# Second routing's logits moved from TensorE to VectorE, Pool and ScalarE in a fused attention and two-layer expert kernel

## The chip, the cores and the metric

The kernel runs on one core of one Trainium2 chip. The metric is the device time of one execution in microseconds (us). The core's engines are TensorE (PE in the rows, its weight loads PEld), VectorE (DVE), ScalarE (ACT), GpSimd (POOL) and SyncE (SP); each runs its own instruction stream, and they meet at semaphores.

## The reference

Causal attention with forgetting, then two expert layers on its output. Each expert layer picks one of 8 experts for each of 2304 rows by the largest logit and scales that expert's output by the winning probability:

```python
# layer 2 (layer 1 takes normalised rows times normalised expert embeddings / tau as logits)
logits = x @ w_gate                      # x: output of layer 1, 2304 x 512; w_gate: 512 x 8
expert_idx = np.argmax(logits, axis=1)
probs = softmax(logits)
gate_w = probs[np.arange(N), expert_idx]
for e in range(E):
    xe = x[expert_idx == e]
    h = np.maximum(xe @ w1[e], 0.0)      # 512 -> 1024
    out[expert_idx == e] = gate_w[...] * (h @ w2[e])   # 1024 -> 512
```

## The kernel before

Attention runs over 32 heads in an order written out by hand. Beside it the first layer's routing is made, which fills a table in device memory: for each expert, in places of 128, the entries (row to gather, row to write, gate weight, place).

Then come two expert layers, m = 0 and m = 1, with the same code. For each expert a loop runs over its tiles of 128 rows (here 21 tiles in layer 0: experts have 2, 3, 3, 3, 2, 2, 3 and 3; 23 in layer 1). Each engine has its own copy of the loop, `tile_body`. All products are made in three passes, with high and low parts: hi by hi, hi weights' rest `wlo` by hi, and hi by the input's rest. One tile is:

- Pool gathers the rows (`rows_of`, L1212), TensorE turns them (L566), ScalarE makes `xT_hi` (L732), VectorE `xT_lo` (L1040). This runs one tile ahead.
- TensorE makes h in two halves (L559, 12 matmuls of 512 columns each). ScalarE does the first relu (L723) and the second (L728), TensorE turns h (L564, L572), ScalarE makes `hT_hi` (L730, L734), VectorE `hT_lo` (L1072, L1077).
- TensorE makes y (L588, 24 matmuls). VectorE copies the rows' numbers (`y_idx`, L1088) and scales y into `y_s` (L1089), and Pool stores it (`store_y`, L1228).

In an expert's first tile (`split`) ScalarE and VectorE also split the eight chunks of the next expert's weights, `whi` (L655, 128x1024) and `wlo` (L982), for the other of two buffers. They stand in two groups or more in the order of the tile: chunks 0 and 1, chunk 2 and up to 4, then 5 to 7.

Layer 0 also makes the second routing, for the y of the tile before. TensorE turns `y_s` (L570), ScalarE copies that to `xrT` (L650), TensorE makes the eight logits (L424, L581) and later the ranks (`ranks1`, L427). VectorE picks the expert (`route_choose`, L880, L886 to L904), ScalarE takes the exponentials (`route_exp`), and VectorE makes the entries of the table of layer 1 (`route_enter`, L910 to L927), which Pool scatters (`store_entries`, L1237). `link` (L757) makes VectorE wait for its own last instruction.

Every order is that of the code; a `wait_ge` stops its engine and everything behind it there. Pool's stream in a tile is: the next entries, their gather, the store of y, the store of the entries.

## Time and profile before

| | |
|---|---|
| median of 3 runs | 945.73 us (944.29 to 945.82) |
| the profiled execution | 944.56 us |
| its span, first to last instruction | 943.0 us |
| mean granted TensorE clock | 0.968 |
| busy: PE, PEld, DVE, ACT, POOL | 878.1, 722.4, 555.7, 403.5, 291.1 us |
| layer 0, first relu of the first to that of the last tile | 335.49 to 616.96 us |

The span is that of the profiled execution; the rows of its trace give starts in us from the span's beginning. Busy time of an engine that isn't waited for costs nothing, so what counts is the chain that sets the distance of one tile to the next.

### The profile page before, as it was taken

The numbers are of one execution on the slowest core, as the hardware profiler recorded it, in microseconds if no ns is written. First come the engines' busy times: TensorE is split into PE (matmuls) and PEld (weight loads), VectorE is DVE, ScalarE is ACT, GpSimd is POOL, SyncE is SP. The second block draws the span as 40 slices with busy tenths as digits, with TensorE's granted clock in tenths as the row PEclk, the third lists the DMA queues.
The fourth block names the chain that finished last, engine by engine and source line by source line (L and its number), as shares of the span: only waits on it lengthen the run. The fifth ranks groups of instructions, "written<-read, shape, count | busy, mean of one in ns | idle before, by whom it ended". The sixth has DMA issues, their size and how long they took to land.

```text
span 943.0 us, 16443 instructions
## 1 busy us (share of the span) xinstructions
PE 878.1 (93%) x5092; PEld 722.4 (77%) x5093; DVE 555.7 (59%) x1667; ACT 403.5 (43%) x708; POOL 291.1 (31%) x459
## 2 busy tenths in 40 slices
PE   6999988987988689999999999978999999999996
PEld 5787776766766568888888888867888888888884
DVE  6777674666766257675848874753554162626643
ACT  2554552553555045352625652614443242425542
POOL 6444334344332523222322322313212221122211
PEclk7999997998999899999999999999999999999998
DMA  4444442453530184543516642602565142616100
GB/s 130 112 116 114 123 119 64 142 160 95 143 111 13 29 299 163 177 136 115 184 59 213 213 170 86 216 20 90 197 216 184 46 150 102 211 46 217 39 30 23
DMA packets 59244, 119.64 MB, mean 127 GB/s; under 512 B 11934, under 2 KB 20638, under 8 KB 59204
## 3 DMA queue, kind: packets, MB, share of 16 engines
q1 hardware_dynamic: 49476, 96.90, 32.2%
q0 software_dynamic: 9440, 22.18, 7.2%
q8 instruction: 20, 0.33, 0.1%
q14 instruction: 20, 0.16, 0.1%
q10 hardware_dynamic: 288, 0.07, 0.0%
HBM read 104.14 MB, written 17.99 MB: 130 GB/s over the span
## 4 chain that ended last, share of the span: by engine, by line
PE 84%; DVE 4%; ACT 4%; DMA 3%; issue 2%; POOL 2%; SPq 1%; another core or an unknown queue 0%; POOLq 0%; DVEq 0%; ACTq 0%
PE ps L588 26%; PE ps L559 25%; PE ps L406 8%; PE ps L419 7%; PE ps L414 4%; PE ps L377 2%; PE ps L378 2%; PE ps L389 2%; PE ps L390 2%; PE ps L447 2%; PE ps L424 2%; ACT o_rows L638 1%; DMA xg<-x,ent_next 1%; PE ps L396 1%; DMA k_raw<-in_k 1%
## 5 line engine op out<-in xcount | busy, mean ns | idle before, releaser
L982 DVE TENSOR_TENSOR wlo<-stage,whi 128x1024 fp32r<-128x1024 f32 x136 | 160.0, 1220 | 31.6 <-ACT whi L655 26.0
L655 ACT CAST whi<-stage 128x1024 fp32r<-128x1024 f32 x136 | 133.7, 1055 | 0.1
L406 PE MATMUL ps<-probT,v_s 128*65 128x448 f32 (+4 forms) x384 | 109.2, 409 | 12.5 <-POOL probT L1143 12.4
L723 ACT ACTIVATE h_s<-ps 128x512 f32<-128x512 f32 x44 | 26.3, 599 | 220.5 <-PE ps L559 218.6
L823 DVE CUSTOM_DVE_ANT_0 ps<-ps,maskf 128x576 f32<-128x576 f32 (+4 forms) x160 | 76.1, 508 | 51.6 <-PE ps L378 51.6
L588 PE MATMUL ps<-whi,hT_hi 128*128 128x512 f32 x352 | 100.5, 408 | 0.0
L588 PE MATMUL ps<-whi,hT_lo 128*128 128x512 f32 x352 | 99.2, 403 | 0.0
L559 PE MATMUL ps<-whi,xT_hi 128*128 128x512 f32 x352 | 95.1, 392 | 3.0 <-DVE xT_lo L1040 3.0
L588 PE MATMUL ps<-wlo,hT_hi 128*128 128x512 f32 x352 | 95.2, 393 | 0.0
L559 PE MATMUL ps<-whi,xT_lo 128*128 128x512 f32 x352 | 95.1, 392 | 0.0
L559 PE MATMUL ps<-wlo,xT_hi 128*128 128x512 f32 x352 | 94.7, 391 | 0.0
L624 ACT ACTIVATE probT<-ps 128x576 f32<-128x576 f32 (+4 forms) x160 | 66.2, 435 | 53.1 <-PE ps L390 49.3
L389 PE MATMUL ps<-qB,kB 97*128 97x288 f32 (+2 forms) x192 | 72.4, 385 | 10.6 <-ACT probT L624 10.6
L559 PEld LDWEIGHTS ps<-whi,xT_hi 128*128 128x128 f32 x352 | 65.7, 188 | 18.1 <-ACT xT_hi L714 3.5
L588 PEld LDWEIGHTS ps<-wlo,hT_hi 128*128 128x128 f32 x352 | 66.6, 189 | 14.9
L559 PEld LDWEIGHTS ps<-wlo,xT_hi 128*128 128x128 f32 x352 | 66.1, 188 | 14.6
L559 PEld LDWEIGHTS ps<-whi,xT_lo 128*128 128x128 f32 x352 | 66.1, 188 | 14.4
L1072 DVE TENSOR_TENSOR hT_lo<-ps,hT_hi 128x512 fp32r<-128x512 f32 x44 | 30.4, 690 | 73.1 <-ACT hT_hi L730 72.9
L588 PEld LDWEIGHTS ps<-whi,hT_hi 128*128 128x128 f32 x352 | 63.3, 190 | 11.3
L588 PEld LDWEIGHTS ps<-whi,hT_lo 128*128 128x128 f32 x352 | 63.0, 188 | 11.7
L406 PEld LDWEIGHTS ps<-probT,v_s 128*65 128x65 f32 x384 | 47.1, 143 | 28.8 <-issue 17.0
L1216 POOL COPY ent_next<-ent_tab 128x4 int32 (+1 forms) x46 | 8.5, 186 | 193.5 <-DVE ent_mid L1041 191.6
(188 smaller groups left out, 1582.3 us busy)
## 6 DMA issues: line engine op xcount, KB each, us to landing
stage<-in_moe_w SPq DMA_DIRECT2D x128, 512.0 KB, 3.7
q_raw<-in_q SPq DMA_DIRECT2D x64, 144.0 KB, 3.1
k_raw<-in_k SPq DMA_DIRECT2D x64, 144.0 KB, 3.1
v_s<-in_v SPq DMA_DIRECT2D x32, 162.5 KB, 2.2
x<-o_rows SPq DMA_DIRECT2D x8, 512.0 KB
kB<-cum_hl SPq DMA_DIRECT2D x64, 2.2 KB, 1.8
table<-entry POOLq DMA_INDIRECT x44, 2.1
table<-tinit SPq DMA_DIRECT2D x2, 288.0 KB
```

What stands on the lines that cost most here:

```text
L389: pe.matmul(o, kB[a][0:ROW + 1, k0:k0 + P], qB[a][0:ROW + 1, lo:hi], start=True, stop=False)
L406: mm = pe.matmul(ps[0:D + 1, OT_AT + lo:OT_AT + hi], v_s[h % 3][:, t, :], probT[:, col:col + hi - lo], start=(t == 0), stop=(t == QT - 1 o ...
L414: mm = pe.matmul(back_ps[:, t, :], o_t[:, t * P:(t + 1) * P], i_emb[:, h % H, :], start=True, stop=True)
L419: mm = pe.transpose(bank[:, c * P:(c + 1) * P], src[:, c * P:(c + 1) * P], ident[:])
L559: mm = pe.matmul(h_ps[hf], x[:, c * P:(c + 1) * P], w1_sl(w[b], c, hf * 512, 512), start=(wi == 0 and c == 0), stop=(wi == 2 and c == DC - 1))
L588: mm = pe.matmul(y_ps, h[:, kk * P:(kk + 1) * P], w2_sl(w[b], kk), start=(hf == 0 and wi == 0 and kk == 0), stop=(hf == 1 and wi == 2 and ...
L624: act.activation(probT[0:M, PT_AT[t]:PT_AT[t] + S - t * P], ps[0:M, T_AT[t]:T_AT[t] + S - t * P], ACT.Exp, scale=-1.0).then_inc(exps_done, 1)
L655: act.copy(whi[b][:, c, :], stage[:, c, :]).then_inc(w_hi[c], 1)
L723: act.activation(h_s[:, 0:512], h_ps[0], ACT.Relu).then_inc(h_relu[0], 1)
L823: dve.tensor_tensor_reduce(out=tile, in0=tile, in1=maskf[0:M, at:at + q1], scale=1.0, scalar=LARGE, op0=ALU.add, op1=ALU.min, accum_out=sm ...
L982: dve.tensor_tensor(wlo[b][:, c, :], stage[:, c, :], whi[b][:, c, :].bitcast(F32), ALU.subtract).then_inc(w_lo[c], 1)
L1072: dve.tensor_tensor(hT_lo[:, 0:512], hT_ps[0], hT_hi[:, 0:512].bitcast(F32), ALU.subtract).then_inc(h_lo[0], 1)
```

## The change

In layer 0 the turn of `y_s`, the copy `xrT` and the eight logits on TensorE go. The logits come from products of `y_s` with the gate's rows, which a new input brings broadcast over all partitions (`wg_rows`, 128 x 8 x 512, loaded by SP before head 16). For experts 0 to 2 VectorE multiplies and sums (`first_logits`); for 3 to 7 Pool multiplies (`products`) into two buffers in turn, and ScalarE sums (`accumulate`). The scale of y goes from VectorE to ScalarE and waits for `y_placed`, the copy of `y_idx`. On VectorE the entries of a tile's choice are made one tile later, ahead of the next choice, with `ent_prev` for the rows' numbers, and so the ranks on TensorE too, between the two halves of h. In split tiles ScalarE splits chunks 0 and 1 ahead of the first relu, not behind it. After the last tile the last logits are still made on TensorE, as before, and there is one pass of entries more. Layer 1 is as it was.

```diff
@@ TensorE, tile
                                 mm.then_inc(h_done[hf], 1)
+                                if m == 0 and hf == 0:
+                                    pe.wait_ge(oh_done, tile.get(1, B - 1))
+                                    ranks1().then_inc(rank_done, 1)
                             yr = tile.get(1, 1 + 2 * m)
                             pe.wait_ge(y_ready, yr)
-                            if m == 0:
-                                turn_rows(y_s, yT_ps).then_inc(r_turned, 1)
...
-                                    if wi == 2 and m == 0 and hf == 0:
-                                        pe.wait_ge(rT_ready, tile.get(1, 1))
-                                        pe.wait_ge(ent_done[1], tile.get(1, 1))
-                                        logits(wg_s, rt_lg).then_inc(logits_done, 1)
-                                    if wi == 2 and m == 0 and hf == 1:
-                                        pe.wait_ge(oh_done, tile.get(1, B))
-                                        ranks1().then_inc(rank_done, 1)
@@ ScalarE
+            def accumulate(i, k):
+                act.wait_ge(prod_done, k)
+                act.activation(prod[i % 2][:], prod[i % 2][:], ACT.Copy,
+                               accum_out=lg[:, 0, NV + i:NV + i + 1]).then_inc(acc_done, 1)
...
                 act.copy(xT_hi[:], x_ps).then_inc(x_hi, 1)
+                if m == 0:
+                    for i in range(NP):
+                        accumulate(i, i + 1)
@@ ScalarE, tile
+                            if split and m == 0:
+                                for c in range(0, 2):
+                                    split_hi(1 - b, c, nw)
                             act.wait_ge(h_done[0], n)
                             act.activation(h_s[:, 0:512], h_ps[0], ACT.Relu).then_inc(h_relu[0], 1)
...
+                            if m == 0:
+                                for i in range(2):
+                                    accumulate(i, tile.get(NP, i + 1))
                             act.wait_ge(h_done[1], n)
                             act.activation(h_s[:, 512:1024], h_ps[1], ACT.Relu).then_inc(h_relu[1], 1)
...
                             if m == 0:
-                                route_turned(tile.get(1, 1), yT_ps)
+                                for i in range(2, NP):
+                                    accumulate(i, tile.get(NP, i + 1))
...
                                 route_exp(tile.get(1, B))
+                                act.wait_ge(y_done, n)
+                                act.wait_ge(y_placed, n)
+                                act.activation(y_s[:], y_ps, ACT.Copy,
+                                               scale=ent_cur[:, 2:3].bitcast(F32)).then_inc(y_ready, 1)
@@ VectorE
+            def first_logits():
+                for i in range(NV):
+                    ins = dve.tensor_tensor_reduce(out=yT_ps, in0=y_s[:], in1=wg_rows[:, i, :], scale=1.0, scalar=0.0,
+                                                   op0=ALU.mult, op1=ALU.add, accum_out=lg[:, 0, i:i + 1])
+                    link(ins)
@@ VectorE, tile
                             if split:
                                 for c in range(0, 2):
                                     split_lo(1 - b, c, nw)
+                            if m == 0:
+                                first_logits()
...
+                            if m == 0:
+                                route_enter(rank_n, ex_n, out_n, one_rk, one_ent)
+                                link(dve.tensor_copy(ent_rt[:], ent_prev[:]))
                             if split:
                                 split_lo(1 - b, 2, nw)
                             if m == 0:
-                                route_choose(1, tile.get(), one_rt)
+                                dve.wait_ge(acc_done, acc_n)
+                                route_choose()
                             if split:
                                 for c in range(3, 5):
                                     split_lo(1 - b, c, nw)
...
+                            if m == 0:
+                                dve.wait_ge(y_out, out_n)
+                                dve.tensor_copy(y_idx[:], ent_cur[:, 1:2]).then_inc(y_placed, 1)
@@ Pool
+            def products(n):
+                for i in range(NP):
+                    pool.wait_ge(acc_done, tile.get(NP, 1 - NP + n) if i == 0 else tile.get(NP, i - NP + n))
+                    pool.tensor_tensor(prod[i % 2][:], y_s[:], wg_rows[:, NV + i, :], ALU.mult).then_inc(prod_done, 1)
...
                             store_y(m, tile.get(1, 2 * m) if m else n)
                             if m == 0:
+                                products(0)
                                 store_entries(n)
```

ScalarE, an expert's first tile in layer 0, before. `h_s` is the relu, `ISA` stands for waits on a register.

```order
L723 ACTIVATE h_s<-ps 128x512
L654 ISA
L655 CAST whi<-stage 128x1024 x2
L728 ACTIVATE h_s<-ps 128x512
L730 CAST hT_hi<-ps 128x512
```

And now, from the split of chunks 0 and 1 to the second relu:

```order
L657 CAST whi<-stage 128x1024 x2
L731 ACTIVATE h_s<-ps 128x512
L242 ISA
L651 ACTIVATE prod,lg<-prod 128x512
L242 ISA
L651 ACTIVATE prod,lg<-prod 128x512
L739 ACTIVATE h_s<-ps 128x512
```

Two sums now stand between the two relus, and the two splits ahead of the first.

The end of the same tile on ScalarE, now, from the third sum on:

```order
L651 ACTIVATE prod,lg<-prod 128x512
L657 CAST whi<-stage 128x1024 x3
L242 ISA
L646 ACTIVATE ex<-lgm 128x8
L756 ACTIVATE y_s<-ps,ent_cur 128x512
L657 CAST whi<-stage 128x1024 x3
```

The scale of y, which waits for VectorE, stands ahead of the last three splits.

Pool, one tile, now (before, only the copy, the two DMAs and the DMA of the entries stood there):

```order
L1264 COPY ent_next<-ent_tab 128x4
L239 ISA
L1272 DMA xg<-x,ent_next 128x512
L1281 DMA y<-y_s,y_idx 2305x512
L242 ISA
L1289 TENSOR_TENSOR prod<-y_s,wg_rows 128x512
L242 ISA
L1289 TENSOR_TENSOR prod<-y_s,wg_rows 128x512
```

The products (five in all, the last three follow in the same way) stand between the store of y and that of the entries.

## Rows read from the trace of the kernel before

**Rows 1.** Waits, 330 to 640 us: who waited for whom, total, times, longest.
```profile
POOL y L1233 <- DVE y_s L1089: 111.3, 21, 11.4
```

**Rows 2.** ScalarE's first relus in order of time: start, duration, idle before.
```profile
335.49 0.60 ACT L723 ACTIVATE h_s<-ps 128x512 f32<-128x512 f32 x1 [3.90 <-PE ps L559]
...
353.98 0.60 ACT L723 ACTIVATE h_s<-ps 128x512 f32<-128x512 f32 x1 [3.00 <-PE ps L559]
...
616.96 0.60 ACT L723 ACTIVATE h_s<-ps 128x512 f32<-128x512 f32 x1 [5.84 <-PE ps L559]
...
675.51 0.60 ACT L723 ACTIVATE h_s<-ps 128x512 f32<-128x512 f32 x1 [7.63 <-PE ps L559]
...
687.95 0.60 ACT L723 ACTIVATE h_s<-ps 128x512 f32<-128x512 f32 x1 [1.96 <-PE ps L559]
```

**Rows 3.** TensorE in order of time, an ordinary tile of layer 0.
```profile
403.45 1.07 PE L588 MATMUL ps<-whi,hT_hi 128*128 128x512 f32 x4
...
404.36 1.08 PE L588 MATMUL ps<-wlo,hT_hi 128*128 128x512 f32 x4
...
406.37 1.12 PE L559 MATMUL ps<-whi,xT_hi 128*128 128x512 f32 x4
```

**Rows 4.** Groups of VectorE by form: count, busy us, mean ns, idle before.
```profile
L823 DVE CUSTOM_DVE_ANT_0 ps<-ps,maskf 128x448 f32<-128x448 f32 x32 | 20.4, 639 | 9.6 <-PE ps L378 9.5
L823 DVE DVE_READ_ACCUMULATOR2_ANT smin<- 128x1 fp32r x128 | 18.0, 141 | 0.0
```

**Rows 5.** ScalarE in order of time, activations with accumulator.
```profile
111.92 0.62 ACT L638 ACTIVATE o_rows<-o_rows 128x512 f32<-128x512 f32 x1
...
112.53 0.62 ACT L638 ACTIVATE o_rows<-o_rows 128x512 f32<-128x512 f32 x1
```

**Rows 6.** Pool in order of time, a copy.
```profile
248.38 0.66 POOL L1136 CAST kB<-kA 64x576 fp32r<-64x576 f32 x1 [4.43 <-DVE kA L783]
```

**Rows 7.** Pool and VectorE in order of time, a copy beside a two-input instruction.
```profile
242.36 1.16 POOL L1131 CAST qB<-qA 64x576 fp32r<-64x576 f32 x1 [0.27 <-ACT qA L618]
...
242.25 0.75 DVE L795 TENSOR_TENSOR kA<-k_raw,kB 64x576 fp32r<-64x576 f32 x1
```

**Rows 8.** In order of time, layer 1's first tile from the second relu.
```profile
653.39 0.60 ACT L728 ACTIVATE h_s<-ps 128x512 f32<-128x512 f32 x1 [0.26 <-PE ps L559]
...
654.52 1.20 PE L588 MATMUL ps<-whi,hT_hi 128*128 128x512 f32 x4
...
655.77 0.68 DVE L1077 TENSOR_TENSOR hT_lo<-ps,hT_hi 128x512 fp32r<-128x512 f32 x1
```

**Rows 9.** VectorE in order of time: entries, the next tile, an expert's first tile.
```profile
393.58 0.16 DVE L914 COPY entry<-ent_rt 128x2 int32<-128x2 int32 x1
...
396.11 0.17 DVE L1067 COPY ent_cur<-ent_mid 128x4 int32<-128x4 int32 x1 [0.56 <-DVE ent_rt L1093]
...
411.14 0.17 DVE L1067 COPY ent_cur<-ent_mid 128x4 int32<-128x4 int32 x1 [1.77 <-issue]
```

**Rows 10.** In order of time, the middle of an expert's first tile.
```profile
415.91 1.23 DVE L982 TENSOR_TENSOR wlo<-stage,whi 128x1024 fp32r<-128x1024 f32 x1 [0.24 <-ACT whi L655]
...
417.05 0.15 DVE L886 TENSOR_SCALAR valid<-ent_rt 128x1 f32<-128x1 int32 x1
...
417.82 2.93 ACT L655 CAST whi<-stage 128x1024 fp32r<-128x1024 f32 x3
...
418.70 2.35 DVE L982 TENSOR_TENSOR wlo<-stage,whi 128x1024 fp32r<-128x1024 f32 x2
```

**Rows 11.** In order of time, the scale of y and Pool's store of it.
```profile
406.76 0.74 DVE L1089 TENSOR_SCALAR y_s<-ps,ent_cur 128x512 f32<-128x512 f32 x1
...
408.36 1.01 POOL L1233 DMA_INDIRECT y<-y_s,y_idx  x1 [5.18 <-DVE y_s L1089]
```

**Rows 12.** Layer 0's first tile: TensorE's turn of the gathered rows, then a window.
```profile
341.47 0.66 PE L419 MATMUL ps<-ident,xg 128*128 128x128 f32 x4 [2.83 <-DMA xg<-x,ent_next]
...
343.00:345.00 2.00, 2.00 (x7) 1.61 (x7) 1.24 (x3) 1.54 (x3) 0.28 (x2) 0.50 1.04 408
```

More of the change, by code:

```diff
@@ L40, in attention_moe_moe @@
     HALF = H // 2
+    NV = 3
+    NP = E - NV
     SCALE = -float(D) ** -0.5
@@ L166, in attention_moe_moe @@
         y_idx = sb("y_idx", [P, 1], I32)
+        ent_prev = sb("ent_prev", [P, 4], I32)
+        prod = [sb(f"prod{a}", [P, DM]) for a in range(2)]
+        wg_rows = sb("wg_rows", [P, E, DM])
         ps = ctx.enter_context(nc.psum_tensor("ps", [P, 8 * 512], F32))
@@ L317, in _ @@
             for h in range(HEADS):
+                if h == 2 * H:
+                    sp.dma_start(wg_rows[:].rearrange("p e d -> p (e d)"), wg_t).then_inc(wg_in, 16)
                 if h + 2 < HEADS:
@@ L420, in turn_rows, with logits @@
                 return mm
-            def logits(w, o, rows=xrT):
+            def logits(w, o, rows):
                 for c in range(DC):
@@ L706, in _ @@
                 else:
-                    act.wait_ge(ent_out, tile.get(16, 32))
+                    act.wait_ge(ent_out, tile.get(16, 48))
                     act.wait_ge(tab_in[0], 16 * E // 2)
@@ L748, in _ @@
                 if m == 0:
-                    route_turned(tile.get(1, 1), yT_ps)
+                    act.wait_ge(r_turned, 1)
+                    act.copy(prod[0][:], yT_ps).then_inc(rT_ready, 1)
                     route_exp(tile.get(1, B))
@@ L894, in route_choose @@
                 link(dve.tensor_reduce(first_i[:, lo:lo + g], e, AX.X, ALU.min))
-                if m == 0:
-                    link(dve.tensor_tensor(first_i[:, lo:lo + g], first_i[:, lo:lo + g], pad_row[:], ALU.add))
-                    dve.tensor_tensor(oh[:, lo:lo + g, :], e, wide(first_i, lo, g), ALU.is_equal).then_inc(oh_done, 1)
-                else:
-                    dve.tensor_scalar(oh[:, 0, :], e[:, 0, :], first_i[:, 0:1], valid[:, 0:1], ALU.is_equal,
-                                      ALU.mult).then_inc(oh_done, 1)
@@ L901, in route_choose @@
-                dve.tensor_scalar(region[:, lo:lo + g], first_i[:, lo:lo + g], float(TOK), float(E * TOK), ALU.mult, ALU.add)
-                if m == 1:
-                    link(dve.tensor_scalar(inval[:], valid[:], -float(OOB), float(OOB), ALU.mult, ALU.add))
-                    dve.tensor_tensor(region[:, 0:1], region[:, 0:1], inval[:], ALU.add)
+                link(dve.tensor_tensor(first_i[:, lo:lo + g], first_i[:, lo:lo + g], pad_row[:], ALU.add))
+                dve.tensor_tensor(oh[:, lo:lo + g, :], e, wide(first_i, lo, g), ALU.is_equal).then_inc(oh_done, 1)
@@ new lines, in route_choose_batch, with route_choose @@
+                dve.tensor_scalar(region[:, lo:lo + g], first_i[:, lo:lo + g], float(TOK), float(E * TOK), ALU.mult, ALU.add)
+            def route_choose():
+                l, e = lg[:, 0:1, :], eqi[:, 0:1, :]
+                dve.tensor_scalar(valid[:], ent_rt[:, 3:4], float(E * TOK), None, ALU.is_lt)
+                link(dve.tensor_reduce(mx[:, 0:1], l, AX.X, ALU.max))
+                link(dve.tensor_tensor(e, l, wide(mx, 0, 1), ALU.is_equal))
+                dve.tensor_tensor(lgm[:, 0:1, :], l, wide(mx, 0, 1), ALU.subtract).then_inc(lgm_done, 1)
+                link(dve.scalar_tensor_tensor(out=e, in0=e, scalar=-float(E), in1=iota8[:].unsqueeze(1), op0=ALU.mult,
+                                              op1=ALU.add))
+                link(dve.tensor_reduce(first_i[:, 0:1], e, AX.X, ALU.min))
+                dve.tensor_scalar(oh[:, 0, :], e[:, 0, :], first_i[:, 0:1], valid[:, 0:1], ALU.is_equal,
+                                  ALU.mult).then_inc(oh_done, 1)
+                dve.tensor_scalar(region[:, 0:1], first_i[:, 0:1], float(TOK), float(E * TOK), ALU.mult, ALU.add)
+                link(dve.tensor_scalar(inval[:], valid[:], -float(OOB), float(OOB), ALU.mult, ALU.add))
+                dve.tensor_tensor(region[:, 0:1], region[:, 0:1], inval[:], ALU.add)
@@ L1278, in _ @@
                     if m == 0:
+                        if late == 0:
+                            products(0)
                         store_entries(tile.get(1, late))
@@ L1281, in _ @@
                     store_entries(tile.get(1, 2))
+                    store_entries(tile.get(1, 3))
             pool.wait_ge(y_out, tile.get(16, 48))
@@ L1306 @@
     }
+    gate = np.asarray(inputs['moe2_w_gate'])
     for name in ('moe_w1', 'moe_w2', 'moe2_w_gate', 'moe2_w1', 'moe2_w2'):
         laid_out[name] = np.asarray(inputs[name])
+        if name == 'moe2_w_gate':
+            laid_out['gate_rows'] = np.broadcast_to(gate.T.reshape(1, -1), (P, gate.size))
     arrays, args = {}, []
```

89 lines of the change are left out of this document (47 added, 42 removed).

## The prediction

> **What bounds the kernel now.** Start with the page's busy shares and the waits of the first expert layer. TensorE is busy almost without a break, and the large waits there are those of others for it or for what follows it: Pool stands 111 us for y_s [rows 1]. Next come the starts of the first relu. The first layer's 20 intervals are one of 18.49 and 19 of 13.84 (353.98 to 616.96); in the second layer they are 12.44 [rows 2]. A tile of the first layer is a tile of the second plus the turn of y, the logits and the ranks. TensorE sets both periods, so removed TensorE work is worth its full time until something else takes longer than the shorter tile.
>
> **What leaves TensorE.** The two periods differ by 1.40. The rank matmuls stay. Two groups of four matmuls with the ranks between them take 2.01 (404.36 to 406.37), where one group alone takes 0.91 [rows 3]; so the ranks cost 0.19. The rest, 1.21 a tile, goes. TensorE alone could run a tile in 12.6.
>
> **What each new step costs.**
> - Three multiply-and-sum instructions on VectorE. The same custom instruction takes 0.64 at 448 wide [rows 4], about 0.70 at 512; with its accumulator read (0.14, mostly overlapped) and the wait that links each to the next I take 0.9. Three are 2.7 a tile.
> - Five sums on ScalarE. A 512-wide activation with accumulator starts 0.61 to 0.62 after the one before [rows 5]. Five are 3.1, and the y scale adds 0.5 to 0.6, while the xrT copy of that size goes.
> - Five products on Pool. No row shows this. One 576-wide copy of one SBUF operand takes 0.66 [rows 6], or 0.58 at 512: the lower bound. Two operands through that rate are 1.15, which I take; the copy that ran beside a two-input VectorE instruction took 1.16 [rows 7], so a product can reach 1.8 with such a delay. On this price alone a page has more: the Trainium skill, "GPSIMD Engine Reference", section 3.1, measures 2.6 cycles an element at 1.2 GHz for a two-tensor add, from which I would estimate 1.1 us, and no run here shows it.
>
> **The new ring.** These steps are harmless only if they stay off the path, and the order written out doesn't let them. ScalarE does the second relu, which TensorE needs for its turn of h and thus for all of the second product, only after sums 0 and 1. These need Pool's products 0 and 1, which come after Pool's store of the last y, which waits for ScalarE's scale, which waits for VectorE's y_idx. And y_idx now stands behind the three logits, the entries, all five sums and the choice. I count from the start of one second relu to the next.
>
> *Ordinary tile.* The second layer shows the second hT_lo on VectorE 2.38 after the relu (653.39 to 655.77), for 0.68 [rows 8]. The entries took 1.98 (393.58 to the end of the 0.37 copy before the idle of 0.56) [rows 9]: 5.2 with a short wait. The choice took 1.65 (417.05 to 418.70) [rows 10], less about 0.1 for the lg copy that goes: 6.8. y_idx 0.15: 7.0. TensorE has y done at 1.13 + 6 x 0.91 + 0.3 = 6.9 [rows 8], so y_idx is last, by a little. ScalarE's scale: 7.6. Pool starts its store 0.86 after y_s and takes 1.01 [rows 11]: 9.5. Two products and gaps of 0.35: 12.15. Sum 1: 12.8. So with no collision 12.8 stands against TensorE's 12.6 and today's 13.84. The three logits run from about 8.0 to 10.7, and product 0 starts at 9.8; if they collide it costs up to 0.7, and at an expert's end Pool also loads a table (up to 1). I take 13.6, between 12.6 and 14.2.
>
> *Into an expert's first tile.* ScalarE must walk the loop's head, where VectorE showed 1.77 of idle time [rows 9] (ScalarE's own was hidden; I take 1.7), then split two chunks before the first relu, 0.98 each (2.93 for three) [rows 10]: 7.6 + 1.7 + 1.96 = 11.3. First relu 0.5, two sums 1.24: 13.0. VectorE's two wlo chunks run from about 10.3 to 12.6, in front of the logits. If product 1 has to wait for them, 14.4.
>
> *Out of that tile.* This is the costly one. VectorE: wlo 0 and 1 end near -0.4 (against the relu), logits 2.3, hT_lo and xT_lo 4.4, entries 6.4, wlo 2 (1.2) 7.6, choice 9.1, wlo 3 and 4 (2.35 [rows 10]) 11.4, y_idx 11.6. Today y_idx stands behind wlo 4 too, but with no logits and no entries ahead of it, and ScalarE doesn't wait for it. Now ScalarE stands before its scale until 11.6, with splits 5 to 7 queued behind: 0.5 + 2.95 gives 15.05; then first relu and two sums, 16.8. TensorE, which wanted the relu at 12.6, idles about 4 us. Pool is worse off if it collides: y_s at 12.2, store to 14.0, and product 0 at 14.3 meets wlo 6 and 7. With two products behind them it is 19 to 20.3.
>
> So the pair of intervals around a first tile takes 13.0 + 16.8 = 29.8 with no collision, 14.4 + 20.3 = 34.7 with all, against 27.7 now. The rows show one such collision: a Pool copy that takes 0.66 alone took 1.16 when a VectorE tensor_tensor with two SBUF inputs started 0.11 before it [rows 7]. The wait was partial, and who goes first isn't shown. I take the middle, 32.2: +4.5.
>
> The Trainium skill says more than the row ("SBUF — State Buffer", section "Who interferes with whom"): a VectorE instruction with two SBUF inputs and a Pool instruction that reads SBUF exclude each other for the whole instruction, by order of issue. By it the sum would be nearer 34.7, and it speaks against giving both engines products of y at once.
>
> **Start, end, and what is free.** At the start Pool's first round of products is on a zero y, and products 2 to 4 wait for ScalarE's sums, which come after xT_hi. So the second gather goes out about 4 later, into full DMA engines. TensorE already waited 2.83 for it, and ran at half of its clock, 0.50, behind that [rows 12]. I take +6 (3 to 8). At the end there is one more pass of entries, 2.0, partly beside TensorE's work: +1.5 (0 to 3). The 2 MB load of wg_rows stands in SP's queue at head 16, ahead of head 18's operands, two heads early; I cost it at nothing, and up to 3 if that cover is gone. Gathers go out after product 4, some 3 us later than now; behind the first tile TensorE waits for no gather in this layer, so I cost that at nothing, and at up to 2 a tile if the cover is less than that. The ranks, moved between the halves of the first product, read a choice made one tile ago: nothing. Each long idle of TensorE may cost 1 to 1.5 in clock, as in rows 12, up to +10 in all; that is for the range.
>
> **Sum.** 7 pairs x 4.5 = +31.5; 5 ordinary intervals x -0.24 = -1.2; start +6; end +1.5: +37.8. The profiled execution took 944.56, 1.17 less than the median of 945.73; 944.56 + 37.8 + 1.17 is 983.5, and I say 983.
>
> **Rivals.**
> 1. Collisions cost nothing and Pool is quick: pairs 29.8 (+14.7), ordinary 12.8 (-5), start +4: 959. For it: the partial wait in rows 7. Chance 0.2.
> 2. Every collision is a full wait, as the page says: pairs 34.7 (+49), ordinary 14, start and end +8: 1003. Chance 0.2.
> 3. Faster: products and sums are always ready, TensorE sets the tile, 19 x -1.21 with +3 at the start: 926. It decides at y_idx of a first tile: that would have to stand some 4 us earlier than I have it. Against it are VectorE's rows, which sum to 11 us without a gap. But ordinary tiles could gain, and first tiles lose less than I think: 0.12.
> 4. The two cancel, within 0.2%: 0.03.
>
> My forecast, part of the collisions, has 0.45. The range of 950 to 1006 takes in rivals 1 and 2 and leaves out the third. A measurement can tell about 0.2% here: faster 0.12, same 0.03, slower 0.85.
>
> **What would show it.** In the changed profile, starts of the first relu should alternate: about 17 to 18 behind an expert's first tile, 13 to 14 elsewhere. ScalarE should wait for y_idx in first tiles, and TensorE for h_s. A Pool product should take 1.1 to 1.2 alone and longer beside wlo. If TensorE's turn of h never waits, I am wrong and it is rival 3; if products take 0.6, rival 1.

## The result, and the profile after

The changed kernel takes 1074.34 us (median of 4 runs, 1071.67 to 1075.73) against 945.38 for the kernel before (median of 4, 944.29 to 945.82): a ratio of 1.136, 95% interval 1.134 to 1.139. The forecast was 983, in a range of 950 to 1006. The direction was right, the size was not: +129 us, where +38 was forecast.

The page of the kernel after, with its busy shares, the chain of work that ended last, and four of its groups (line, engine, operation, count, then busy us, mean ns, idle before it and what ended that):

```profile
PE 919.4 (86%) x4842; PEld 735.6 (68%) x4843; DVE 707.5 (66%) x1787; ACT 479.0 (45%) x928; POOL 449.5 (42%) x570
...
PE 51%; DVE 19%; issue 15%; ACT 6%; POOL 4%; DMA 3%; SPq 1%; DVEq 1%; ACTq 1%; POOLq 0%
...
L1008 DVE TENSOR_TENSOR wlo<-stage,whi 128x1024 fp32r<-128x1024 f32 x136 | 218.9, 1653 | 45.4 <-ACT whi L657 44.7
L1289 POOL TENSOR_TENSOR prod<-y_s,wg_rows 128x512 f32<-128x512 f32 x110 | 159.2, 1475 | 18.0 <-ACT prod L651 17.4
L586 PE MATMUL ps<-whi,hT_lo 128*128 128x512 f32 x352 | 109.0, 436 | 48.1 <-DVE hT_lo L1110 48.0
...
L1001 DVE CUSTOM_DVE_ANT_0 ps<-y_s,wg_rows 128x512 f32<-128x512 f32 x63 | 84.2, 1336 | 1.9
```

TensorE's share fell from 93% to 86%, and TensorE now waits 48 us for `hT_lo`, a wait that it did not have. A `wlo` of 128x1024 took 1.23 in the rows of before [rows 10]; its mean is now 1.65 us, over all 136. The logits' instruction (L1001) has a mean of 1.34, where alone it takes 0.70.

ScalarE's first relus, the rows that answer to [rows 2], are those of the layer's first tile, the next two, its last tile and the first of layer 1:

```profile
343.82 0.59 ACT L731 ACTIVATE h_s<-ps 128x512 f32<-128x512 f32 x1
...
368.17 0.59 ACT L731 ACTIVATE h_s<-ps 128x512 f32<-128x512 f32 x1
...
386.82 0.59 ACT L731 ACTIVATE h_s<-ps 128x512 f32<-128x512 f32 x1
...
741.10 0.60 ACT L731 ACTIVATE h_s<-ps 128x512 f32<-128x512 f32 x1 [2.06 <-PE ps L564]
...
781.83 0.60 ACT L731 ACTIVATE h_s<-ps 128x512 f32<-128x512 f32 x1 [3.91 <-PE ps L564]
```

Three differences hold all of it. The first relu came 8.3 us later than before (335.49). The stretch from it to the last tile's, which I call **the stretch** from here on, is 397.3 us where it was 281.5: +115.8. From there to layer 1's first relu it is 40.7 instead of 33.7: +7.0. Together +131.1, and the two profiled executions differ by 131.2 (1075.73 and 944.56). Layer 1's period is 12.4 in both. The layer's first interval needs care: it was 18.49 before and is 24.35 now, and in the kernels of the experiments it lies anywhere between 16.7 and 25.3. Without it the stretch is 263.0 before and 372.9 now, +110.0.

Inside the stretch the 20 intervals alternate as forecast, but all of them are long. Out of an expert's first tile they are 22.3 to 22.8 (the very first 24.35), ordinary ones 18.5 to 18.8. Into a first tile they are 16.0 to 16.4 behind an expert of three tiles and 18.6 to 19.5 behind one of two.

The waits of the kernel after from 330 to 760 us (who waited for whom, us in total, times, longest):

```profile
ACT ex L646 <- DVE lgm L916: 101.3, 21, 6.1
...
PE ps L586 <- DVE hT_lo L1110: 48.0, 15, 4.9
...
ACT y_s L756 <- DVE y_idx L1130: 28.9, 13, 3.1
PE ps L426 <- ACT h_s L739: 26.9, 17, 2.5
...
DVE entry L934 <- DMA table<-entry: 16.5, 7, 5.0
```

The two waits that I had forecast are there: `y_s` for `y_idx`, and the turn of h for the second relu (L426 for L739). The largest of TensorE's is a third, for `hT_lo`, which stood in no step of mine. Where it comes from is seen in order of time, first in an ordinary tile, then in an expert's first tile:

```profile
427.94 5.63 DVE L1001 CUSTOM_DVE_ANT_0 ps<-y_s,wg_rows 128x512 f32<-128x512 f32 x1
427.98 5.03 POOL L1289 TENSOR_TENSOR prod<-y_s,wg_rows 128x512 f32<-128x512 f32 x4
...
443.53 6.30 DVE L1008 TENSOR_TENSOR wlo<-stage,whi 128x1024 fp32r<-128x1024 f32 x1 [0.54 <-ACT whi L657]
443.79 4.96 POOL L1289 TENSOR_TENSOR prod<-y_s,wg_rows 128x512 f32<-128x512 f32 x4
...
455.08 2.07 PE L586 MATMUL ps<-whi,hT_lo 128*128 128x512 f32 x4 [4.91 <-DVE hT_lo L1110]
...
456.95 1.91 PE L586 MATMUL ps<-whi,hT_hi 128*128 128x512 f32 x4
```

One instruction of VectorE that needs 0.70 lasts 5.63 while Pool runs four products in 5.03, and one that needs 1.2 lasts 6.30. Each has a record that starts ahead of the first product's. VectorE is let in only when Pool stands still, waiting for a sum of ScalarE's. Everything that is queued on VectorE behind it comes late, `hT_lo` among it. TensorE, done with its two passes on `hT_hi`, waits 4.91 us for that, and its next groups of four matmuls take 2.07 and 1.91 us where they take 1.1 to 1.2 at full clock. The granted clock is 0.50, the lower of TensorE's two levels (1.2 of 2.4 GHz), from 455 to 459 us, behind that wait, and 1.00 again from 461. From 353 to 629 us its mean is 0.85, and 1.00 before.

In the layer's second tile it is otherwise. A `wlo` had begun 0.96 us ahead of the first product, it took its 1.23, and then the two engines went by turns:

```profile
366.40 1.23 DVE L1008 TENSOR_TENSOR wlo<-stage,whi 128x1024 fp32r<-128x1024 f32 x1 [1.75 <-ACT whi L657]
367.36 1.39 POOL L1289 TENSOR_TENSOR prod<-y_s,wg_rows 128x512 f32<-128x512 f32 x1
...
368.72 2.24 POOL L1289 TENSOR_TENSOR prod<-y_s,wg_rows 128x512 f32<-128x512 f32 x1
...
369.76 2.28 DVE L1008 TENSOR_TENSOR wlo<-stage,whi 128x1024 fp32r<-128x1024 f32 x1
```

Of the 21 rows of products from the layer's first tile to its last, 13 shut an instruction of VectorE out and 8 went by turns. Whether an instruction is shut out depends on who came first, if Pool's coming is put about 0.74 us ahead of where its record starts. Nine kernels of this document have rows of Pool instructions that read SBUF: this one and those of experiments 3, 4, 7 to 10, 12 and 13. In them 391 VectorE instructions with two SBUF inputs start within 1.2 us ahead of the first record of a row or just with it. All 140 that start at most 0.73 us ahead are shut out. None of the 241 that start 0.745 us or more ahead lasts longer than alone. Of the 10 between, 3 are shut out. In the 8 rows with turns a `wlo` was still running when the first product's record started, and that product took 1.39 to 1.46: there Pool was the one that had to wait first.

### The profile page after: what moved, and what is told of

Read it like the earlier page. It is cut to its first block, busy times and chain, and to the rows that moved or that the text cites. A ratio compares the mean times of both kernels' runs of the same rounds, so it can differ in the third digit from the quotient of the medians.

```text
span 1074.1 us, 16623 instructions
## 1 busy us (share of the span) xinstructions
PE 919.4 (86%) x4842; PEld 735.6 (68%) x4843; DVE 707.5 (66%) x1787; ACT 479.0 (45%) x928; POOL 449.5 (42%) x570
## 4 chain that ended last, share of the span: by engine, by line
PE 51%; DVE 19%; issue 15%; ACT 6%; POOL 4%; DMA 3%; SPq 1%; DVEq 1%; ACTq 1%; POOLq 0%
PE ps L586 16%; PE ps L564 12%; PE ps L413 7%; DVE wlo L1008 7%; PE ps L421 3%; PE ps L426 3%; POOL prod L1289 2%; PE ps L384 2%; ACT whi L657 2%; PE ps L385 2%; PE ps L396 2%; DMA table<-entry 2%; PE ps L397 2%; DVE ps L1001 1%; ACT o_rows L638 1%
## 5 line engine op out<-in xcount | busy, mean ns | idle before, releaser
L1008 DVE TENSOR_TENSOR wlo<-stage,whi 128x1024 fp32r<-128x1024 f32 x136 | 218.9, 1653 | 45.4 <-ACT whi L657 44.7
L1289 POOL TENSOR_TENSOR prod<-y_s,wg_rows 128x512 f32<-128x512 f32 x110 | 159.2, 1475 | 18.0 <-ACT prod L651 17.4
L586 PE MATMUL ps<-whi,hT_hi 128*128 128x512 f32 x352 | 121.2, 475 | 0.0
L586 PE MATMUL ps<-wlo,hT_hi 128*128 128x512 f32 x352 | 106.9, 430 | 0.0
L651 ACT ACTIVATE prod<-prod 128x512 f32<-128x512 f32 x110 | 69.4, 635 | 51.6 <-POOL prod L1289 51.2
L426 PE MATMUL ps<-ident,h_s 128*128 128x128 f32 x352 | 59.3, 295 | 37.4 <-ACT h_s L739 26.9
L586 PEld LDWEIGHTS ps<-wlo,hT_hi 128*128 128x128 f32 x352 | 77.0, 219 | 19.6
L586 PEld LDWEIGHTS ps<-whi,hT_hi 128*128 128x128 f32 x352 | 76.8, 229 | 15.3
L1001 DVE CUSTOM_DVE_ANT_0 ps<-y_s,wg_rows 128x512 f32<-128x512 f32 x63 | 84.2, 1336 | 1.9
L426 PEld LDWEIGHTS ps<-ident,h_s 128*128 128x128 f32 x352 | 42.3, 149 | 53.9 <-issue 31.2
```

The costliest lines, as they stand in the source:

```text
L426: mm = pe.transpose(bank[:, c * P:(c + 1) * P], src[:, c * P:(c + 1) * P], ident[:])
L586: mm = pe.matmul(y_ps, h[:, kk * P:(kk + 1) * P], w2_sl(w[b], kk), start=(hf == 0 and wi == 0 and kk == 0), stop=(hf == 1 and wi == 2 and ...
L651: act.activation(prod[i % 2][:], prod[i % 2][:], ACT.Copy, accum_out=lg[:, 0, NV + i:NV + i + 1]).then_inc(acc_done, 1)
L1001: ins = dve.tensor_tensor_reduce(out=yT_ps, in0=y_s[:], in1=wg_rows[:, i, :], scale=1.0, scalar=0.0, op0=ALU.mult, op1=ALU.add, accum_out= ...
L1008: dve.tensor_tensor(wlo[b][:, c, :], stage[:, c, :], whi[b][:, c, :].bitcast(F32), ALU.subtract).then_inc(w_lo[c], 1)
L1289: pool.tensor_tensor(prod[i % 2][:], y_s[:], wg_rows[:, NV + i, :], ALU.mult).then_inc(prod_done, 1)
```

## The experiments

The measure is the time and, since parts of the computation are left out in some kernels (which changes the tiles of layer 1), the stretch. All but the twelfth have one execution each. The kernel before took 943 to 950 us beside them, and the first interval of the stretch moves by some us from kernel to kernel, so differences of a few us prove little.

**Theory A:** Pool's products keep VectorE out of a resource that both need to reach SBUF, for a whole row of products, and that is what the time went to. **Theory B:** the new orders do it, the ring from y through products, sums and choice back to the scale of y, whatever Pool's instructions are.

**1. Pool busy as long, but it only writes.**

```diff
-                    pool.tensor_tensor(prod[i % 2][:], y_s[:], wg_rows[:, NV + i, :], ALU.mult)
+                    pool.memset(wide_prod[i % 2][:], 0.0)        # 128x1370
```

> Each of Pool's five products per tile is replaced by a memset of 1370 columns into the same buffer (about 1.25 us by the size, as a product alone): Pool is busy as long and signals as often, but reads nothing from SBUF. The logits of experts 3 to 7 are therefore zero sums and layer 1's tiles differ, so layer 0 is judged by the stretch from the first to the last first relu (281.5 us before, 397.3 after); wg_rows holds three experts only. Theory A (Pool's tensor_tensor products, run back to back, keep VectorE's two-input instructions out; hT_lo comes late, TensorE waits and its clock falls): the stretch falls to about 310 us (295 to 330), no wlo or logits instruction is longer than 1.6 us for one of its size, and TensorE's waits for hT_lo (48 us) fall under 10. Theory B (the longer ring itself: Pool's time, the sums between the relus, the scale of y behind the exponential): the stretch stays within 15 us of 397, since Pool's times and all orders are the same.

Measured: 1046.64 us, stretch 348.4. The line of `wlo` and that of the memsets in this kernel (count, then shortest/median/longest in ns):

```profile
L1009 DVE TENSOR_TENSOR wlo<-stage,whi x136: 1215/1219/1227, 247.1 to 1038.9; 128x1024 fp32r<-128x1024 f32 x136
...
L1291 POOL MEMSET prod<- x110: 1240/1257/1279, 328.3 to 694.4; 128x1370 f32 x110
```

No `wlo` is lengthened any more, though 38 of layer 0's 64 stand beside a memset, and TensorE's waits for `hT_lo` fall from 48.0 to 4.2 us in all. The stretch is 48.9 us shorter. Both theories missed the number: A is right on the cause of the long instructions, but what is left is 67 us above before, not 30.

**2. No Pool work.** The memsets have one column.

> Pool's products are one-column memsets, so Pool's time goes too, and all signals, sums and orders stay (logits of experts 3 to 7 are zero sums; layer 0 is judged by its stretch of relus). Theory A: as the kernel with write-only products, 295 to 325 us, at most 10 us under it, since Pool's time alone is hidden. Theory B with Pool's time in the ring: well under the kernel with write-only products, by 20 us or more. If it is the orders on ScalarE and VectorE that cost, it stays above 360.

Measured: 1014.80 us, stretch 319.1, so 29.3 less than with the long memsets. That is more than the 10 of theory A and what B had asked for (20 or more). It does not tell Pool's time in the ring from a hold by its writes, which experiments 5 and 14 show. Of the 115.8 us, 78.2 go with Pool's work and 37.6 stay: these are the orders. The wait of `entry` for the store of the tile before, right ahead of the choice and of `y_idx`, is now 45.7 us in 22 times: 1.5 to 3.0 each, and 5.1 once, behind the last tile.

**3. The whole changed kernel with an early scale.**

```diff
@@ ScalarE, tile
-                                route_exp(tile.get(1, B))
                                 act.wait_ge(y_done, n)
                                 act.wait_ge(y_placed, n)
                                 act.activation(y_s[:], y_ps, ...)
                             if split:
                                 for c in range(5, CH):
                                     split_hi(1 - b, c, nw)
+                            if m == 0:
+                                route_exp(tile.get(1, B))
@@ VectorE, tile: y_idx and y_placed right behind the second hT_lo, ahead of route_enter
```

> The full changed kernel with the copy of the rows' numbers right behind the second hT_lo on VectorE, and with ScalarE's scale of y ahead of the exponential and the splits of chunks 5 to 7 ahead of the exponential too. Theory A: the products are still there and still shut VectorE out for whole runs; they only start earlier, so the stretch of layer 0 stays between 375 and 400 us (397.3) and the time between 1050 and 1077. Theory B (the late scale closes a ring y, products, sums, choice): the scale moves up by 3 to 4 us a tile, the stretch falls under 345 us and the time under 1025.

Measured: 1046.28 us, stretch 384.0: 13.3 less, inside A's range for the stretch and far from B's. The time gains 28 and falls below A's range for it, because this execution also reached its first relu 13.5 us earlier (below) and lost 2.8 less between the layers.

**4. The other way round: the kernel before, with products that nobody needs.**

```diff
                             store_y(m, tile.get(1, 2 * m) if m else n)
                             if m == 0:
+                                for i in range(5):
+                                    pool.tensor_tensor(out5[i][:], dum[0][:], dum[1][:], ALU.mult)
                                 store_entries(n)
```

> The kernel before, with five tensor_tensor products of 128x512 on Pool in each tile of layer 0 behind the store of y, on tiles that nobody else uses and with nobody waiting for them; all of the computation is as before. Theory A: VectorE's two-input instructions (wlo, hT_lo, xT_lo) are kept out by up to 6 us a tile; the stretch of layer 0 grows from 281.5 to between 305 and 345 us and TensorE waits for hT_lo. Theory B: Pool has the time free (its busy share is low), nobody waits, the stretch stays under 285 us.

Measured: 1067.35 us, stretch 395.5. Nothing but these products was added, no engine waits for them, and they cost 114.0 us of stretch: as much as the whole change. VectorE's group of `scum`, the running sum of the choices, in layer 0 (busy us, mean ns), and one tile in order of time:

```profile
L928 DVE TENSOR_TENSOR scum<-scum,oh 128x8 bf16<-128x8 bf16 x20 | 126.3, 6314 | 0.0
...
438.56 6.99 DVE L928 TENSOR_TENSOR scum<-scum,oh 128x8 bf16<-128x8 bf16 x1
...
439.23 6.28 POOL L1278 TENSOR_TENSOR out<-dum 128x512 f32<-128x512 f32 x5
...
450.84 2.07 PE L590 MATMUL ps<-whi,hT_lo 128*128 128x512 f32 x4 [4.12 <-DVE hT_lo L1074]
```

An addition of 8 columns that takes 0.15 lasts 6.99, from 0.67 us ahead of the first product's record to the end of the fifth. TensorE's wait of 4.12 and its slow matmuls behind it (2.07, 1.91 and 1.64 for groups of 1.1 to 1.2, at a granted clock of 0.50 from 450.8 to 454.8 us) make 6.4 of the 6.9 by which this tile is longer than 13.83. B falls as the main cause, and A stands, but not with its number or its instructions: it had 305 to 345, and `wlo`, `hT_lo` and `xT_lo` kept out. `wlo` keeps its 1.22 here and `hT_lo` its 0.69; the one shut out is tiny, and they stand behind it.

**5 and 6. The early scale, with Pool only writing, and with no Pool work.**

> Write-only Pool work (memsets of 1370 columns in place of the products, so the logits of experts 3 to 7 are zero sums and layer 0 is judged by its stretch of relus) together with the early scale of y. Reads of the products were worth 48.9 us of that stretch (397.3 against 348.4) and the early scale 13.3 us (397.3 against 384.0). If the two add up, it is 335 us. If the early scale was worth so little only because the kept-out VectorE set the tile (theory A), it is worth more here, 25 to 45 us: 303 to 323 us. If the late scale never mattered, 345 to 350.

> One-column memsets in place of the products (logits of experts 3 to 7 are zero sums) together with the early scale: what is left is the order on ScalarE and VectorE alone. The stretch of layer 0 was 319.1 us with the late scale. If the late scale and the entries' wait ahead of it cost the pairs, 285 to 295 us (tiles of 12.4 to 14.4); if the two early splits, the sums between the relus and VectorE's longer row do, it stays over 305 us.

Measured: 1050.53 us with a stretch of 350.3, and 997.77 us with 302.6. The fifth missed: no gain at all over the first (348.4), though the sixth shows that the early scale has something to give. With the scale earlier the memsets stand beside the choice, and its last steps now last as long as a row of memsets. In order of time:

```profile
357.47 4.88 DVE L922 TENSOR_SCALAR oh<-eqi,first_i,valid 128x8 bf16<-128x8 f32 x1
357.53 4.79 POOL L1291 MEMSET prod<- 128x1370 f32 x4
```

So Pool's writes shut VectorE out too, but other instructions of it; experiment 14 comes back to this. The sixth lies between its two readings, nearer to the second: the early scale is worth 16.5 us when nothing is in VectorE's way (319.1 to 302.6).

**7. One SBUF input on Pool in place of two:** in the fourth kernel, `pool.tensor_copy(out5[i][:], dum[:])` of 128x1024.

> The kernel before with five copies of 128x1024 (one SBUF input) on Pool per tile of layer 0 in place of the five added products, about 1.2 us each; all of the computation is as before. With products one tiny two-input instruction of VectorE (scum, L928, 128x8) took 6.3 us a tile. Theory A1 (any Pool instruction that reads SBUF keeps it out): again 5 to 7 us a tile there, the stretch of layer 0 between 380 and 400 us. Theory A2 (only Pool instructions with two inputs): L928 takes under 1.5 us and the stretch is under 290 us.

Measured: 1022.50 us, stretch 356.5. The copies take 1.04 us each, and `scum` has this group:

```profile
L928 DVE TENSOR_TENSOR scum<-scum,oh 128x8 bf16<-128x8 bf16 x20 | 91.3, 4563 | 0.0
```

A copy shuts VectorE out like a product (median of `scum` 5.65 us, and five copies last 5.0). The stretch is under my 380; that the row is 1.3 us a tile shorter explains most of it.

**8. A memset of 300 columns behind each product.**

> The kernel before with the five added products per tile, each followed by a write-only memset of 300 columns (about 0.3 us) on Pool; both inputs of a product are one tile; all of the computation is as before. If the waiting VectorE instruction gets in as soon as no reading Pool instruction runs, scum (L928) takes 0.2 to 1.8 us instead of 6.3 and the stretch of layer 0 falls from 395.5 to under 310 us. If VectorE is let in only when Pool stops or after a fixed number, it takes 5 us or more and the stretch stays over 375 us.

Measured: 1060.44 us, stretch 393.7. One row of the spaced kernel, in order of time:

```profile
437.64 6.88 DVE L929 TENSOR_TENSOR scum<-scum,oh 128x8 bf16<-128x8 bf16 x1
438.31 1.05 POOL L1278 TENSOR_TENSOR out<-dum 128x512 f32<-128x512 f32 x1
439.29 0.36 POOL L1279 MEMSET gap<- 128x300 bf16 x1
...
444.44 0.34 POOL L1279 MEMSET gap<- 128x300 bf16 x1
```

A memset as such does not stop `scum`: in experiment 14 it stands as close ahead of a row of memsets (0.63 to 0.68 us in 18 of 19 tiles) as here ahead of the products, and keeps its 0.15. Yet gaps of 0.35 us with memsets in them let nothing in. While instructions follow each other on Pool, it keeps the way.

**9. A pause behind each product:** Pool waits for its own product before it issues the next.

```diff
                                     pool.tensor_tensor(out5[i][:], dum[0][:], dum[1][:], ALU.mult).then_inc(pch, 1)
                                     chain.add()
+                                    pool.wait_ge(pch, chain.get())
```

> The kernel before with the five added products per tile, and behind each of them Pool waits for its own product to be done before it issues the next, so that it stands still for a part of a microsecond, in which a memset stood in the spaced kernel. All of the computation is as before. If the port is handed over only when Pool has nothing under way, scum (L928) now gets in behind the first or second product and takes 1 to 3 us instead of 6.3, and the stretch of layer 0 falls from 395.5 to between 282 and 320 us. If VectorE is let in only behind the last of a fixed row of Pool instructions, whatever the gaps, it takes 7 us or more and the stretch is over 390 us.

Measured: 1034.62 us, stretch 362.6. In order of time:

```profile
436.79 2.03 DVE L928 TENSOR_TENSOR scum<-scum,oh 128x8 bf16<-128x8 bf16 x1
437.47 1.32 POOL L1278 TENSOR_TENSOR out<-dum 128x512 f32<-128x512 f32 x1
438.97 1.33 POOL L1278 TENSOR_TENSOR out<-dum 128x512 f32<-128x512 f32 x1 [0.18 <-POOL out L1278]
...
441.92 3.46 DVE L984 TENSOR_TENSOR wlo<-stage,whi 128x1024 fp32r<-128x1024 f32 x2
441.94 2.36 POOL L1278 TENSOR_TENSOR out<-dum 128x512 f32<-128x512 f32 x1 [0.18 <-POOL out L1278]
```

`scum` gets in behind the first product (2.03 us): a pause of 0.18 does what a memset of 0.35 did not. But the stretch gained only 32.9 us, not 75 or more. Two long rows now go by turns: `wlo` has a mean of 1.74 and a product one of 1.57, and Pool's row lasts longer and meets 38 of the layer's `wlo` where in experiment 4 it met one.

**10. The same pause in the changed kernel with the early scale.**

> The changed kernel with the early scale, and Pool waits for each of its products to be done before it issues the next. The whole computation is there. The stretch of layer 0 was 384.0 us with the early scale alone, and 302.6 with the early scale and no products at all. If standing still lets VectorE in, wlo and the logits' instructions take 2.4 us at most and the stretch falls to 320 to 350 us; if Pool's own time in the ring (products, sums, choice) is what is left, the pauses make it longer, 385 to 400 us.

Measured: 1053.68 us, stretch 382.6, so 1.4 less than without the pauses. The longest `wlo` is 2.92 us where it was 6.64, but the mean of the logits' instruction is 1.28 in both. It does not help here: the collisions are cut into pieces, not removed, and my 320 to 350 was wrong.

**11 and 12. Entries staged in a tile of their own**, without products and with them, both with the early scale.

```diff
             def route_enter(n, n_ex, n_out, ranks, ent):
-                dve.wait_ge(ent_out, n_out)
                 dve.tensor_copy(ent[:, 0, 0:2], ...)          # ent is now entry2
...
+                dve.wait_ge(ent_out, n_out)
+                link(dve.tensor_copy(entry1[:], entry2[:]))
                 dve.sem_inc(ent_done[1], 1)
```

> The kernel without products and with the early scale (layer 0: 302.6 us, then 38.8 us to the first relu of layer 1), in which VectorE makes an entry in a tile of its own and copies it into the one that Pool stores only at the end, so that the wait for the store of the tile before comes some 2 us later and at the end of the row. Logits of experts 3 to 7 are zero sums. If this wait (39.5 us in 22 tiles) is on the path, the stretch falls to 285 to 293 us and the stretch between the layers to 33 to 36 us; if not, both stay within 2 us.

> The changed kernel with the early scale and with the staged entries, whole computation, products in place. Without products these two brought layer 0 to 283.7 us; with products and the early scale alone it was 384.0. If the products' hold on the port is what costs, they still cost 80 to 100 us here: 365 to 384 us, and the gap between the layers is about 36 us. If products only cost as long as the other orders are bad, it is under 330 us.

Measured: without products 976.76 us and a stretch of 283.7, 18.9 less than in the sixth kernel. With products 1044.97 us (ratio to before 1.106, interval 1.099 to 1.113) and a stretch of 381.1. So with the orders mended the products cost 97.5 us, more than in the kernel as changed: their price is not the orders' doing. And all of this change with products at no cost (283.7) is not shorter than the kernel before (281.5).

**13. One product per tile on the kernel before.**

> The kernel before with one added product per tile of layer 0 instead of five; all of the computation is as before. Five cost 114 us of the stretch of layer 0 (281.5 to 395.5). If every product has its share of that (scum is kept out for one product, 1.3 us more, and all of it is on the path), the stretch is 295 to 305 us; if VectorE has slack for one, 281 to 286 us.

Measured: stretch 285.4 (time 940.45, with an early first relu). `scum` lasts 2.0 us in most tiles (median 2026 ns), and 3.9 us are lost in 20 intervals. The first of them happens to be 1.8 shorter than before (16.7); the other 19 lose 5.7 us, where with five products they lose 111.8. So five cost some twenty times what one does: VectorE had room for one wait of 1.9, not for one of 6.8.

**14. Memsets on the kernel before.**

> The kernel before with five memsets of 128x1370 (about 1.25 us each) per tile of layer 0 in place of the five added products: Pool writes and reads nothing; all of the computation is as before. Two-input instructions (scum, L928, and wlo) should keep their 0.16 and 1.22 us. If only reads cost, the stretch stays between 281 and 290 us. But in an earlier run copies and tensor_scalars of VectorE grew beside memsets to 5.7 us; if such a one stands there in most tiles (the copy of ent_rt or ent_cur), the stretch is 340 to 395 us as with products.

Measured: 1031.57 us, stretch 374.2, inside the range for the case that a copy stands there. In order of time:

```profile
439.99 0.15 DVE L927 TENSOR_TENSOR scum<-scum,oh 128x8 bf16<-128x8 bf16 x1
...
440.29 6.36 DVE L1094 COPY ent_rt<-ent_cur 128x4 int32<-128x4 int32 x1
...
440.64 5.98 POOL L1272 MEMSET out<- 128x1370 bf16 x5
```

Here it is the copy of 4 columns behind `scum` that lasts 6.36. In the fourth kernel it was `scum`, and the copy behind it, 0.17 us, came when Pool had finished.

## Why the prediction failed, step by step

The direction and the order of the long and short intervals came as forecast. In the forecast's own terms the seven pairs took 40.0 each where it had 32.2 (+85.9 in place of +31.5), and the five ordinary intervals 18.6 where it had 13.6 (+24.1 in place of -1.2). The start is +14.2 in place of +6, the end +7.0 in place of +1.5. One step carries most of it.

- **TensorE's part, right.** Without Pool's work (experiment 2) ordinary intervals are 12.2 to 13.1; I had 12.6 for TensorE alone. No run shows the ring's 12.8 free of collisions with Pool's time in it: with the long memsets an ordinary interval is 14.1.
- **Prices of one instruction, right but for the product.** Three logits start 0.79 apart (426.35, 427.14, 427.94), taken as 0.9. Sums start 0.62 apart (433.10 and 433.72), taken as 0.62. A product takes 1.25 to 1.30 alone, where I took 1.15. The estimate of 1.1 from the Trainium skill, "GPSIMD Engine Reference", section 3.1, was a little lower still. The median of the 105 products in experiment 4 is 1.29.
- **The failed step: what a collision costs.** I wrote of the ordinary tile that the logits run beside product 0 and "if they collide it costs up to 0.7", and I took the middle between no collision and one wait. What stands there is 5.63 for 0.70, +4.9. The step had two faults. It counted the wait of one instruction for one other, where VectorE waits for the whole row of products up to Pool's next pause. And it priced it at the colliding instruction and at Pool, when VectorE's `hT_lo` stands behind it and TensorE's last pass behind that. An expert of three tiles (into, out and an ordinary interval) was forecast at 32.2 + 13.6 = 45.8, and at 48.7 with every collision a full wait. It took 57.3 (16.4, 22.3 and 18.7), 46.8 without Pool's work, 41.5 before. So my second rival failed too, for the same reason: 1003 against 1074.
- **The row it was judged by.** [rows 7] showed one Pool copy that took 1.16 instead of 0.66 beside a VectorE instruction. There Pool was the one that waited, and only one instruction of it stood there: the row could show neither what a series does nor that VectorE can be the one shut out, though I did write that who goes first isn't shown.
- **The published rule.** The Trainium skill, "SBUF — State Buffer", section "Who interferes with whom", has a VectorE instruction with two SBUF inputs and a reading Pool instruction exclude each other for a whole instruction, and has it depend on who issues first. That there is a full block, and that reads make it for `tensor_tensor` and writes do not, is what experiments 1, 4 and 14 show. That the order decides agrees too, with Pool's coming some 0.74 us ahead of its record (140 of 140 and 241 of 241, above). The length does not agree where Pool was first: in these runs it goes on over four and five instructions. I held this rule as a rival only, and even its price of one instruction was far too low.
- **Orders without collisions, too low by 28.** Rival 1, pairs of 29.8 and ordinary intervals of 12.8, makes a stretch of 291 with the first interval as it was; experiment 2 has 319.1. Of the 28, 4.7 are in that first interval and belong to the start; the pairs are 33.3. What I left out is the wait of `entry` for the store of the tile before, 1.5 to 3.0 us in each tile (moved to the end of its row in experiment 11, it gave back 18.9). I had "5.2 with a short wait". The late scale, which I did name, is worth 16.5.
- **Clock.** I let up to 10 us for it in the range and nothing in the sum. In the tile of experiment 4 three groups of matmuls behind the stall of 4.12 took 2.3 us more than at full clock. Were it so in each of 20 tiles it would make 46 us, an estimate of mine from that one tile.
- **Start, +6 forecast, +14.2 measured.** The forecast's start was the late second gather, and that came as told: it goes out 7.4 us after `xT_hi` where it was 2.7, and TensorE waits 5.5 us for it where it was 2.83. It falls into the first interval, which is 5.9 longer. Ahead of it, the first relu came 8.3 later. From `xT_hi` to the first relu it is 8.05 instead of 4.49, so 3.6 is the five sums and two early splits. The other 4.8 arose before, in attention, and can't be laid to the change: in the six kernels made from the kernel before, whose attention is untouched, `xT_hi` came between 321.3 and 336.6 (331.0 before, 335.8 after). Two with the whole load of `wg_rows` (experiments 2 and 6) had it at 330.7 and 330.9, so that load costs nothing that can be seen in this spread.
- **End, +1.5 forecast, +7.0 measured.** The added pass of entries waits for the store of the entries before it to land. In the changed kernel that wait is 5.04 us (at 759.25). From experiment 2, in order of time, the same wait:

```profile
673.25 0.17 DVE L934 COPY entry<-ent_rt 128x2 int32<-128x2 int32 x1 [5.06 <-DMA table<-entry]
```

Staging gave back only 1.8 of it (38.8 to 37.0), less than I expected. Experiment 4, with no added pass, is at 37.0 too, 3.3 above before, with nothing but products. How the 7.0 divides stays open.

What stays open besides: why Pool keeps VectorE out through all of its row where it did not have to wait itself, and goes by turns where its product had to wait for a `wlo`. That tells the two cases apart, but it is not a mechanism. Nor do the runs show whether Pool takes the way 0.74 us ahead of its work or its records start late; the profile calls its spans on Pool rough. In all those rows the instruction ahead of Pool's first product was its store of y, so it may be other behind another one. Why attention ends up to 15 us apart between kernels with the same attention is open too.

## What to carry to other kernels

Before work is given to Pool because it is idle, list VectorE's instructions that fall beside it: with two SBUF inputs if Pool reads, copies and tensor_scalars too if it writes, tiny ones included. Price each by the length of Pool's whole unbroken row, and then follow what is queued behind it on VectorE to the engine that sets the end. One Pool instruction at a time in a place with a microsecond or two of slack can be nearly free; a row of five is not, and pauses only cut it up. The quickest test is the added work alone, with nobody waiting for it, on the kernel before: here it cost 114 us where the whole change costs 116. The two are not parts of one sum, as the orders cost 37.6 without any work of Pool's; but one run was enough to show that the products had no place in this loop.

## What the runs showed of the hardware

- A VectorE `tensor_tensor` with both inputs in SBUF is kept out by reading Pool instructions (products, copies) for their whole row if it starts at most 0.73 us ahead of the row's first record: 0.15 us became 6.99 beside five products. One that starts 0.745 us or more ahead keeps its time. Where such a one still ran when the row's first record started, as a `wlo` did in 8 rows of the changed kernel, the two engines went by turns. With one input in PSUM (`hT_lo`, `xT_lo`) it kept its 0.68 to 0.69 in every kernel.
- Pool's memsets, which read nothing, leave two-input instructions alone (longest `wlo` 1.227 us in experiment 1) and shut out copies and tensor_scalars: 6.36 us for a copy of 128x4 beside five memsets, 4.88 for a tensor_scalar beside four. Products, which read and write, do both: a copy of 128x4 lasted 5.17 us beside four of them in experiment 12.
- Memsets of 0.35 us between products do not let a waiting `tensor_tensor` in, a pause of 0.18 us does.
- VectorE's record of a shut-out instruction starts before Pool's row and counts as busy. In experiment 4 VectorE runs the 1667 instructions of the kernel before and is busy 685.2 us in place of 555.7: a busy engine in such a profile may be one that waits.
